# A gated scan and two feed-forward layers on one core: the first matmul of each layer as seven block products

## The reference

```
f = lb + (1 - lb) * sigmoid(f_logit);  h = f[:, t] * h + (1 - f[:, t]) * x[:, t];  y[:, t] = h    # over t
z   = relu(y @ w_in1)**2 @ w_out1                  # 12160 tokens, 256 -> 2048 -> 256
out = elu(z @ w_in2) @ w_out2                      # elu(h) = h for h > 0, else exp(h) - 1
```

## Time and profile before

| | |
|---|---|
| median of three runs | 2102.64 us |
| the profiled execution: time, span | 2103.11 us, 2101.3 us |
| TensorE: busy, matmuls | 2073.3 us, 9216 |
| VectorE and ScalarE: busy | 1200.7 us and 1204.3 us |
| GpSimd: busy | 48.3 us |
| mean granted clock of TensorE | 0.999 of full |
| moved by DMA | 46.15 MB, 22 GB/s over the span |

### The profile page before, as it was taken

The page is one execution under the profiler, slowest core; times in us unless marked ns, Lnnn a source line. Parts: engine busy times, 40 slices in busy tenths (PEclk is TensorE's granted clock), DMA queues, the critical chain, the costliest instruction groups (busy, mean ns, idle before and its releaser), DMA issues.

```text
span 2101.3 us, 28406 instructions
## 1 busy us (share of the span) xinstructions
PE 2073.3 (99%) x9216; PEld 1725.4 (82%) x9216; DVE 1200.7 (57%) x1928; ACT 1204.3 (57%) x2020; POOL 48.3 (2%) x40
## 2 busy tenths in 40 slices
PE   6999999999999999999999999999999999999998
PEld 5788888888888888888888888888888888888887
DVE  7955646556465564655646556455564655645544
ACT  4465655655556555565555655656556565565655
POOL 4400000000000000000000000000000000000000
PEclk9999999999999999999999999999999999999999
DMA  4411001010010100100101001010010100100000
GB/s 123 95 25 31 21 10 30 1 29 20 10 30 4 26 20 10 30 8 22 24 6 30 12 18 27 2 30 16 14 30 0 30 20 10 25 0 10 1 11 18
DMA packets 179101, 46.15 MB, mean 22 GB/s; under 512 B 172928, under 2 KB 179072, under 8 KB 179072
## 3 DMA queue, kind: packets, MB, share of 16 engines
q1 hardware_dynamic: 178944, 45.79, 9.7%
q0 software_dynamic: 128, 0.00, 0.0%
HBM read 33.29 MB, written 12.45 MB: 22 GB/s over the span
## 4 chain that ended last, share of the span: by engine, by line
PE 96%; DVE 2%; issue 1%; SPq 0%; ACT 0%; DMA 0%; POOL 0%; DVEq 0%; ACTq 0%
PE acc L258 48%; PE up L258 48%; SPq L186 0%; DVE y L514 0%; DVE hid_hi L560 0%; DVE gate L498 0%; DVE x_t L506 0%; DVE x_t L480 0%; DVE win_hi L475 0%; DMA x_raw<-in_x_dram 0%; DVE hid_lo L562 0%; DVE gate L480 0%; DVE wout L475 0%; ACT hid_hi L442 0%; POOL win_lo L641 0%
## 5 line engine op out<-in xcount | busy, mean ns | idle before, releaser
L258 PE MATMUL acc<-hid_hi,wout 128*128 128x512 f32 (+1 forms) x3072 | 1063.5, 387 | 3.3 <-DVE hid_lo L562 2.9
L258 PEld LDWEIGHTS acc<-hid_hi,wout 128*128 128x128 f32 x3072 | 576.3, 188 | 120.1 <-DVE hid_lo L562 4.5
L258 PE MATMUL acc<-hid_lo,wout 128*128 128x512 f32 (+1 forms) x1536 | 594.1, 387 | 0.0
L585 DVE TENSOR_TENSOR hid_lo<-hid,hid_hi 128x512 fp32r<-128x512 f32 (+1 forms) x384 | 263.7, 687 | 519.2 <-ACT hid_hi L442 519.2
L403 ACT ACTIVATE half<-up 128x512 f32<-128x512 f32 (+1 forms) x384 | 227.4, 592 | 439.9 <-PE up L258 439.6
L430 ACT ACTIVATE half<-up 128x512 f32<-128x512 f32 (+1 forms) x384 | 227.9, 593 | 356.4 <-PE up L258 356.2
L258 PEld LDWEIGHTS acc<-hid_lo,wout 128*128 128x128 f32 x1536 | 288.4, 188 | 57.1
L560 DVE CAST hid_hi<-hid 128x512 fp32r<-128x512 f32 (+1 forms) x384 | 160.2, 417 | 304.5 <-ACT hid L413 304.5
L258 PE MATMUL up<-y_hi,win_lo 128*128 128x512 f32 (+1 forms) x800 | 308.9, 386 | 18.3 <-DVE y_lo L527 17.9
L258 PE MATMUL up<-y_lo,win_hi 128*128 128x512 f32 (+1 forms) x800 | 308.5, 386 | 0.0
L258 PE MATMUL up<-y_hi,win_hi 128*128 128x512 f32 (+1 forms) x800 | 308.2, 385 | 0.0
(11 more groups left out here) (32 smaller groups left out, 837.4 us busy)
## 6 DMA issues: line engine op xcount, KB each, us to landing
f_raw<-in_f_logit_dram SPq DMA_DIRECT2D x184, 64.0 KB, 2.0
x_raw<-in_x_dram SPq DMA_DIRECT2D x184, 64.0 KB, 2.0
out_dram<-o_sb SPq DMA_DIRECT2D x184, 64.0 KB, 1.7
stage<-in_moe_w_in_dram SPq DMA_DIRECT2D x32, 64.0 KB
stage<-in_moe_w_out_dram SPq DMA_DIRECT2D x8, 256.0 KB
stage<-in_moe_w_in_dram SPq DMA_DIRECT2D x8, 256.0 KB
stage<-in_moe_w_out_dram SPq DMA_DIRECT2D x32, 64.0 KB
f_raw<-in_f_logit_dram SPq DMA_DIRECT2D x8, 48.0 KB, 1.9
```

Of the source, the lines that this page charges most:

```text
L258: mm = nc.tensor.matmul(out_ap, lhs[a], rhs[b], start=start and t == 0, stop=stop and t == 2)
L585: nc.vector.tensor_tensor(hid_lo[:, (j - 1) % RING, 0:N], hid[:, (j - 1) % 2, 0:N], hid_hi[:, (j - 1) % RING, 0:N].bitcast(F32), ALU.subtr ...
```

## The change

- The block becomes 512 steps of each batch (`S = BANK`), 11 of them and a tail of 448. A phase (one layer of one block) goes through 8 pairs of `d_ff` chunks (`PAIRS`).
- The first matmul of a pair is a 2x2 by 2x2 block product: two chunks by two halves of `d_model` by two batches. It is made as seven products (`ORDER`, m1 to m7) of sums of weight blocks with sums of input blocks, where there were eight. Each is three matmuls as before, into one of four PSUM banks (`ring`). The second matmul is as it was: four hidden tiles by two output halves by three matmuls. A pair has 21 + 24 = 45 matmuls.
- The four hidden tiles of a pair are added up from the seven products. ScalarE copies m1 and m2 out of PSUM; VectorE adds the other five (`u`, then `t`, `x_n0`), GpSimd adds m1 and m2 (L1330). Relu, square, exponential, ELU, rounding and rest are then done on two tiles, 1024 columns, at a time. VectorE's cast of `hid_hi` (L560) goes to ScalarE, the affine part of the gates (L498) as well.
- The input sums of the next phase are made meanwhile: ScalarE rounds (`split_b` to `split_tb`), GpSimd makes four sums and the low parts (`hosted` in its block).
- The weight sums are made once in the first two phases (four sums on GpSimd, high part on ScalarE, low part on VectorE), written to memory (`s_kept`, `w2_kept`), and from then on loaded for each pair: 128 partitions by 7 x 2 x 128 floats (0.92 MB) in two transfers (`load_s`), in layer 2 also the pair's part of `w_out2` (0.52 MB, `load_w2`).
- Scans and turns work on pieces of 256 steps of one batch, placed between the steps of a pair (`hosted`).

```diff
-UP_BANKS = 2
-LAG = 3
-SLOTS = 4
...
+HALF = 256
+PAIRS = 8
...
+ORDER = ("m1", "m2", "m6", "m7", "m5", "m3", "m4")
+SI = {"m1": 0, "m2": 1, "m6": 2, "m5": 3, "m3": 4, "m7": 5, "m4": 6}
+TI = {"m1": 0, "m2": 1, "m3": 2, "m5": 3, "m7": 4, "m4": 5, "m6": 6}
 RING = 4
+NP = 7
+GROUPS = ((0, 3), (3, 7))
...
-    S = BANK // B
+    S = BANK
...
+        s_kept = nc.dram_tensor("s_kept", [2, PAIRS, P, NP * 2 * P], F32, kind="Internal").ap()
+        w2_kept = nc.dram_tensor("w2_kept", [PAIRS, P, 2 * 2 * D], F32, kind="Internal").ap()
...
+        ring = psum("ring", [P, RING, BANK])
+        acc = psum("acc", [P, B, CH, BANK])
...
+            def load_s(pr, q):
+                v = pr.par()
+                lo, hi = GROUPS[q]
+                w = 2 * P
+                if known(pr.phase.order, 1):
+                    sp.wait_ge(s1_stored[v], DMA_INC * PAIRS // 2)
+                if known(pr.phase.order, 2):
+                    sp.wait_ge(s2_stored, DMA_INC * (pr.p + 1))
+                sp.dma_start(s_w[:, v, lo:hi].rearrange("p x h m -> p (x h m)").bitcast(F32),
+                             s_kept[pr.layer - 1, pr.p][:, lo * w:hi * w]).then_inc(s_loaded[v][q], DMA_INC)
...
+            def triple(out_ap, lhs, rhs, start, stop):
+                for t, (a, b) in enumerate(((1, 0), (0, 1), (0, 0))):
+                    mm = nc.tensor.matmul(out_ap, lhs[a], rhs[b], start=start and t == 0, stop=stop and t == 2)
+                return mm
...
+            def step(cur, old):
...
+                if cur is not None:
+                    weights_in(cur, 0)
+                    inputs_in(t_lb)
+                    if not early(cur.g):
+                        pe.wait_ge(u3_done, cur.g)
+                    product("m1", cur).then_inc(m1_done, 1)
+                if old is not None:
+                    down(old, 0, 0)
+                if cur is not None:
+                    inputs_in(t_lbb)
+                    if not early(cur.g):
+                        pe.wait_ge(u4_done, cur.g)
+                    product("m2", cur).then_inc(m2_done, 1)
+                if old is not None:
+                    down(old, 0, 1)
...
+            def step(ph, p):
+                cur, last = pair_of(ph, p), pair_of(ph, p - 1)
+                N, g = cur.N, cur.g
+                hosted(ph, p, "a")
...
+                nc.scalar.activation(m1_sb[:, 0:N], bank("m1", cur), ACT.Copy).then_inc(m1_kept, 1)
+                if last is not None:
+                    n1_of(last)
+                hosted(ph, p, "b")
+                if last is not None:
+                    relu_of_n0(last)
...
+                nc.scalar.activation(xb[:, cur.par(), 0, 0:N], bank("m2", cur), ACT.Copy).then_inc(m2_kept, 1)
+                if last is not None:
+                    act_of_n0(last)
+                    hi_of_n1(last)
+                hosted(ph, p, "c")
+                if last is not None:
+                    hi_of_n0(last)
+                hosted(ph, p, "d")
...
+            def elu_of(pr, v, x2, acted, done):
+                dve.wait_ge(acted, pr.g + 1)
+                nc.vector.scalar_tensor_tensor(out=x2, in0=ee[:, v, :, 0:pr.N], scalar=1.0, in1=x2,
+                                               op0=ALU.subtract, op1=ALU.max).then_inc(done, 1)
+            def lo_of(pr, k, x2, hi, done):
+                N = pr.N
+                dve.wait_ge(hi, pr.g + 1)
+                nc.vector.tensor_tensor(hid_lo[:, pr.par(), k:k + 2, 0:N], x2,
+                                        hid_hi[:, pr.par(), k:k + 2, 0:N].bitcast(F32),
+                                        ALU.subtract).then_inc(done, 1)
...
+            def step(ph, p):
+                cur, last = pair_of(ph, p), pair_of(ph, p - 1)
+                N, g = cur.N, cur.g
+                u = u_sb[:, :, 0:N]
+                if last is not None and last.layer == 2:
+                    elu_of(last, 0, x_n1(last), acted_n1, elu_n1)
...
+                nc.vector.tensor_tensor(u[:, 0], bank("m6", cur), m1_sb[:, 0:N], ALU.add).then_inc(u2_done, 1)
...
+                nc.vector.tensor_tensor(u[:, 1], bank("m7", cur), u[:, 0], ALU.add).then_inc(u3_done, 1)
+                if last is not None and last.layer == 2:
+                    elu_of(last, 1, x_n0(last), acted_n0, elu_n0)
+                hosted(ph, p, "a")
+                if last is not None:
+                    lo_of(last, 0, x_n1(last), hi_n1, lo_n1)
...
+                t = x_n1(cur)
+                nc.vector.tensor_tensor(t, bank("m5", cur).unsqueeze(1).broadcast_to([P, 2, N]), u,
+                                        ALU.add).then_inc(u4_done, 1)
...
+                nc.vector.tensor_tensor(t[:, 0], bank("m3", cur), t[:, 0], ALU.add).then_inc(c12_done, 1)
+                hosted(ph, p, "b")
...
+                nc.vector.tensor_tensor(x_n0(cur)[:, 1], bank("m4", cur), u[:, 1], ALU.add).then_inc(c21_done, 1)
+                if last is not None:
+                    lo_of(last, 2, x_n0(last), hi_n0, lo_n0)
+                hosted(ph, p, "c")
...
+            def hosted(ph, p):
...
+                nxt = second(ph.i - 1) if ph.layer == 1 else None
+                if ph.layer == 2 and not known(ph.i, TAIL):
+                    nxt = second(TAIL) if known(ph.i, TAIL - 1) else first(ph.i + 2)
+                if nxt is None:
+                    return
+                if p == 2:
+                    lo_b(nxt)
+                    sum_t1(nxt)
+                if p == 3:
+                    lo_bb(nxt)
+                    sum_t3(nxt)
+                if p == 4:
+                    sum_t2(nxt)
+                    sum_t4(nxt)
+                if p == 5:
+                    lo_ta(nxt)
+                if p == 6:
+                    lo_tb(nxt)
...
+            def step(ph, p):
+                cur = pair_of(ph, p)
+                N = cur.N
+                t = xb[:, cur.par(), 0, 0:N]
+                pool.wait_ge(m1_kept, cur.g + 1)
+                pool.wait_ge(m2_kept, cur.g + 1)
+                nc.gpsimd.tensor_tensor(t, t, m1_sb[:, 0:N], ALU.add).then_inc(c11_done, 1)
+                hosted(ph, p)
...
```

More of the change, by code:

```diff
@@ L66, in steps_of, with n, first, second @@
         return S_TAIL if known(i, TAIL) else S
[L69 to L76, removed]
+    @dataclass
+    class Phase:
+        layer: int
+        i: object
+        order: object
+        base: object
+        def n(self):
+            return steps_of(self.i)
+    def first(i):
+        if known(i, 0):
+            return Phase(1, 0, 0, 0)
+        return Phase(1, i, 2 * i - 1, PAIRS * 2 * i - PAIRS)
+    def second(n):
+        if known(n, TAIL):
+            return Phase(2, n, LAST, PAIRS * LAST)
+        return Phase(2, n, 2 * n + 2, PAIRS * 2 * n + 2 * PAIRS)
+    def phase_before(ph):
+        if ph.layer == 1:
+            if known(ph.i, 0):
+                return None
+            return first(0) if known(ph.i, 1) else second(ph.i - 2)
+        return second(TAIL - 1) if known(ph.i, TAIL) else first(ph.i + 1)
+    @dataclass
+    class Pair:
+        layer: int
+        g: object
+        k: object
+        p: int
+        N: int
+        phase: Phase
+        def par(self):
+            return self.p % 2
+    def pair_of(ph, p):
+        while p < 0:
+            ph = phase_before(ph)
+            if ph is None:
+                return None
+            p += PAIRS
+        return Pair(ph.layer, ph.base + p, PAIRS * ph.i + p, p, ph.n(), ph)
+    def early(v):
+        return isinstance(v, int) and v <= 0
     with ExitStack() as ctx:
@@ new lines, in phase @@
+            def phase(ph):
+                for p in range(PAIRS):
+                    step(pair_of(ph, p), pair_of(ph, p - 2))
+            phase(first(0))
+            phase(first(1))
+            phase(second(0))
+            phase(first(2))
+            with pe.Fori(1, TAIL - 3) as n:
+                phase(second(n))
+                phase(first(n + 2))
+            phase(second(TAIL - 3))
+            phase(first(TAIL - 1))
+            phase(second(TAIL - 2))
+            phase(first(TAIL))
@@ L605, in _, with phase @@
+            def phase(ph):
+                for p in range(PAIRS):
+                    step(ph, p)
             nc.vector.memset(carry[:, :, :, :], 0.0).then_inc(carried, 1)
-            attention(0, 0)
             dve.wait_ge(lb_loaded, DMA_INC * G)
@@ new lines, in step, with phase @@
+            def step(ph, p):
[6 more added lines that the diff above has]
+                hosted(ph, p)
+            def phase(ph):
+                for p in range(PAIRS):
+                    step(ph, p)
+            for p in range(2):
+                sums(1, p)
+                pool.wait_ge(s_hi, p + 1)
+                nc.gpsimd.tensor_tensor(s_w[:, p % 2, :, 1, :], r_slot(p), s_w[:, p % 2, :, 0, :].bitcast(F32),
+                                        ALU.subtract).then_inc(s_lo_first, 1)
```

1372 lines of the change are left out of this document (933 added, 439 removed).

## The result

The changed kernel takes 2070.42 us (median of 4 runs, 2068.27 to 2072.95), the kernel before, timed beside it, 2102.66 us: ratio 0.9847, 95% interval 0.983 to 0.9864. It is faster by 1.5%. The profiled execution, the fastest of the four, took 2068.27 us with a span of 2066.4 us. The forecast was 2064 us, within 2005 to 2135.

A forecast was written before the change was run, and what follows sets the result against it. TensorE was taken to set the time from 17.89 us on. Terms 1938.7 + 27 + 39 + 46 + 12 gave 2062.7 us of span; adjusted for time around the span and the median, 2064 us, range 2005 to 2135.

The forecast's parts named there:

- matmuls: TensorE's whole run: 7920 matmuls of 512 columns and 720 of 448, at carried-over prices, take 1938.7 us.
- start: Before the third product: VectorE's turns, gates, scans, low parts and sums take 27 us (24 to 33).
- phases 0 and 1: First two phases: making weight sums between steps, layer 2's through one buffer, costs 39 us (20 to 65).
- layer 2: Layer-2 phases: GpSimd holding VectorE costs 4 us a phase beyond slack, 46 us in all (0 to 104).
- layer 1: Layer-1 phases: without the two ELUs on VectorE, the slack covers GpSimd's holds; 0 us.
- end: After the last product: ScalarE and VectorE finish the pair, then the stretch from the last turn; 12 us (8 to 17).
- what the prediction left open: VectorE's additions out of PSUM, five of nine instructions: counted as running free beside GpSimd, though no run showed it.
- the signs of being wrong: Layer-2 phases over 89 or under 83 us, TensorE waiting for weight loads, lengthened PSUM additions, lower mid-run clock, start beyond 33 us.
- the rule on shared inputs: VectorE instructions with two SBUF inputs contend with GpSimd ones reading SBUF; the loser is held for the whole instruction.
- Late weights: Rival: weight loads share one queue with row transfers and come late, +267 us in layer 2; 2285 us, chance 5%.
- VectorE as the bound: Rival: VectorE, held by GpSimd, limits mainly layer 2, costing 122 us instead of 46; 2140 us, chance 20%.
- TensorE as the bound throughout: Rival: layer 2 costs 0 and the first phases 30 us; 2009 us, chance 20%.

The follow-up runs named there:

- the halves: Against the changed kernel, each of GpSimd's three low parts of 1024 columns is made as two instructions of 512; 2033.91 us.
- The eighth product: Against the changed kernel, product m4 of every pair is computed twice, so a pair has 48 matmuls again; 2163.43 us.
- the start's experiment: Against the changed kernel, VectorE makes the gate's two constants after its first turn, and ScalarE waits for them behind its first tanh; 2067.91 us.
- the earlier write: Against the changed kernel, the second phase's write of layer 2's weight sums is issued in the step that made them, ahead of the wait for m4; 2065.23 us.
- the short loads: Against the changed kernel, each load of weight sums moves only the first product's slice (128 KB instead of 512 or 384 KB); 2061.75 us.
- the last kernel: Against the kernel combining halves, earlier write, start edit and moved low part, the second phase's weight rounding and low part come later; 2008.64 us.

## Why the prediction was right, and where it was not

The time is 6.4 us above the forecast, the span 3.7 us above its sum. Term by term (us):

| term | predicted | measured | how read |
|---|---|---|---|
| matmuls | 1938.7 | 1938.7 | 0.2266 each where TensorE runs (1387.5 / 6122 with the halves) |
| start | 27 (24 to 33) | 37.7 | third product's first matmul |
| phases 0 and 1 | 39 (20 to 65) | 43.5 | 88.0 - 70.8 and 107.9 - 81.6 |
| layer 2 | 46 (0 to 104) | 34 | phases against those with the halves |
| layer 1 | 0 | 4 | the same |
| end | 12 (8 to 17) | 8.5 | the rest of the span, not read by itself |

1. *Matmuls.* Right to 0.1%. The eighth product shows it from the other side: 24 more matmuls make a layer-1 phase 5.0 us longer, where the price says 5.4: the missing 0.4 us is the wait of item 3, which they fill.
2. *Layer 2.* The mechanism was right: held instructions on VectorE, TensorE waiting for what stands behind them, additions out of PSUM free (1.21 us beside GpSimd at 1283.73, and 1212 ns on the mean of the middle, against 1225 for this size in the kernel before; of those of 1024 columns between 316 and 1900 us, 57 ran beside GpSimd for half their time or more, and none took over 1.22 us, which answers what the prediction left open). The phase of 84.9 us against 85.6 predicted is the best of the forecasts. Inside, three things were off. The long low part alone takes 2.4 us (guess 2.3). The steps are 10.1, 10.4, 10.0, 10.2, 10.8, 10.4, 11.5 and 11.6: two long ones, where I had four of 11.2 to 11.6. A low part of 1024 columns shows in the step behind it, as 10.8, 11.5 and 11.6; the first of the three costs only 0.6 us, and the step with the last scans takes 10.4 us, not 11.2. And TensorE stands for `hid_lo` itself, as the operand of its second matmul (11.2 us in 21 waits from 316 us on), more than for m5's and m3's additions (2.3 us in 14): I had named the instructions behind the low part and not the reader of the low part.
3. *Layer 1.* I had the slack cover it; 0.4 us a phase is not covered (its last step takes 10.7 us, and 10.3 with the halves, so this too is the long low part).
4. *Start.* The step that failed: 37.7 us against 27 (24 to 33), and a start beyond 33 us was one of the signs of being wrong. The sum counted VectorE's own work from a first turn at 6.53 us. The added 10.7 us, read from the timeline:

```profile
8.89 1.24 DVE L866 STREAM_TRANSPOSE z_raw<-xa 128x1024 f32<-128x1024 f32 x1
...
13.52 0.69 DVE L1161 SCALAR_TENSOR_TENSOR y_raw<-z_raw,y_raw 128x512 f32<-128x512 f32 x1 [2.27 <-ACT z_raw L832]
...
15.03 2.37 POOL L1340 TENSOR_TENSOR s_w<-o_sb,s_w 128x896 fp32r<-128x896 f32 x1 [2.76 <-ACT s_w L650]
15.45 2.50 DVE L1161 SCALAR_TENSOR_TENSOR y_raw<-z_raw,y_raw 128x512 f32<-128x512 f32 x1
...
23.66 0.69 DVE L928 TENSOR_TENSOR t_lo<-y_raw,t_hi 128x512 fp32r<-128x512 f32 x1 [2.07 <-ACT t_hi L837]
...
24.99 2.98 DVE L1166 TENSOR_TENSOR_SCAN y_raw<-z_raw,carry,y_raw 128x512 f32<-128x512 f32 x1
```

   The first turn is 2.4 us later; GpSimd's low parts of weights hold one gate and one scan for 1.8 and 1.7 us; VectorE is idle for ScalarE for 2.3, 2.1 and 1.2 us (1.28 us of the first is the table's load, shown with the start's experiment). That is 11.5 us, less some 0.2 us for each of four scans (1.28 us, I had 1.5). I had applied the rule on shared inputs to the middle and not to the start, and added up one engine's work where two hand over to each other.
5. *Phases 0 and 1.* Phase 0 exact (88.0), but only in sum: its steps take 8.1, 8.9, 14.8, 11.1, 12.8, 10.6, 12.7 and 9.0 us, where I had 8, three of 12, 11.5 and three of 10.8. Phase 1 is 3.9 us short. The cause given (one buffer, write late) is one of several: the earlier write alone brings the phase to 105.1 us, with the halves, the start and the low part moved it is 95.2, with the rounding moved 88.4. Two causes were missing: the wait's place on ScalarE ahead of m2's copy, and 5.3 us in which TensorE waits for a low part that GpSimd makes only behind weight sums, which wait for a transfer.
6. *Rivals.* Late weights: out by the short loads. VectorE as the bound: out, since with the halves it does the same work and TensorE never stands. TensorE as the bound throughout (2009 us): not this kernel, but the best version measured here ends there, at 2008.64.

That the total came so near is in good part luck, since the errors were of both signs: +10.7 and +4.5 and +4 against -12 and -3.5, 35 us in all where the sum is off by 3.7. What isn't luck is the price of the matmuls and the phase of layer 2.

## What to carry to other kernels

When a change hands an idle GpSimd elementwise work, price it by what it holds up on VectorE: cut its instructions so that none holds VectorE longer than the slack of the step; here that alone was worth 36 of the 39 us that its input sums and low parts cost. Follow what stands behind a waiting instruction on its own engine: reordering alone (a write, a rounding, a low part, two constants) took 25 us out of start and second phase. A start is a chain of hand-overs between engines: walk it instruction by instruction and don't add up one engine, and look where a wait stands in front of the load of ScalarE's table.

## What the runs showed of the hardware

- GpSimd alone takes 0.46 us for a two-input instruction of 128 columns, 1.28 to 1.30 us for 512 and 2.35 to 2.40 us for 1024: hardly a fixed part, and twice VectorE's 1.22 us for 1024.
- An instruction that is held is recorded with its wait: 3.42 us for 1.22 us of work. The one that was issued earlier goes first, and the holder keeps the inputs for its whole length. With the halves VectorE got in between two GpSimd instructions in a row. The Trainium skill ("SBUF — State Buffer", Who interferes with whom) says that issue order decides who is blocked, for the whole instruction; the rows agree.
- In the first two phases the changed kernel has four stretches with matmuls 0.43 us apart, the lower level of 1.2 GHz, each behind a stand of TensorE; but not each stand has one behind it. Two of nearly the same length:

```profile
161.88 0.74 PE L447 MATMUL ring<-t_hi,s_w 128*128 128x512 f32 x1 [2.94 <-ACT xb L808]
...
162.84 0.63 PE L447 MATMUL ring<-t_hi,s_w 128*128 128x512 f32 x1
163.26 0.63 PE L447 MATMUL acc<-hid_hi,wout 128*128 128x512 f32 x1
...
200.82 0.50 PE L447 MATMUL ring<-t_hi,s_w 128*128 128x512 f32 x1 [2.62 <-ACT xb L808]
...
201.39 0.40 PE L447 MATMUL ring<-t_hi,s_w 128*128 128x512 f32 x1
201.62 0.40 PE L447 MATMUL acc<-hid_hi,wout 128*128 128x512 f32 x1
```

  The idle times before the four low stretches are 2.3, 2.7, 5.3 and 2.9 us; before four stands without one they are 2.2 to 2.6 us. The granted clock is 0.96 and 0.97 on the mean of the two phases, against 1.00 in the middle: an estimate from that is up to 3.5 us lost over 87.9 us and up to 3.2 in the second phase. It differs between executions of one kernel: over the whole span it was 0.997 in the profiled one and 0.993 to 0.995 in the other three, which took 2 to 5 us longer. In the last kernel's trace it is 0.98 and 1.00 in the two phases. The very first matmuls, up to 42 us, are 0.43 us apart as well, though the profile's clock reads 1.00 there.
- Writing 0.92 MB of weight sums took 6.5 us (median) beside the full loads and 4.2 us beside the short ones, in a phase where the DMA engines were busy for 78% and 61%.
